# Packing with products for pairs of heads, loads per pair, a split moved into the softmax, and another order of q's turns, in a fused attention and feed-forward kernel on one core

## What is computed

```python
def sm_attn(qq, kk, vv):
    s = scale * np.matmul(qq, kk.transpose(0, 1, 3, 2))
    s = s - np.max(s, axis=-1, keepdims=True)
    a = np.exp(s)
    a = a / (np.sum(a, axis=-1, keepdims=True) + 1e-09)
    return np.matmul(a, vv)
p_packed = sm_attn(p, k, v)
out = sm_attn(q, p_packed, p_packed)
# x = out as (4608, 512); then
h = x @ w_in                       # 512 to 1024
solu = h * softmax(h)
ln = (solu - mean(solu)) / sqrt(var(solu) + 1e-06) * g_ln
x = ln @ w_out                     # 1024 to 512
h = maximum(maximum(x @ w1, x @ w2), x @ w3)
return h @ w_out2
```

## Time and profile before

| | |
|---|---|
| median of three runs | 1071.45 us (1068.35 to 1072.98) |
| profiled execution | 1070.61 us |
| its span, first to last instruction | 1068.8 us |
| mean granted TensorE clock | 0.977 of full speed |
| TensorE busy | 1014.4 us, 95% |
| VectorE, ScalarE, GpSimd busy | 605.5, 344.5, 250.8 us (57%, 32%, 23%) |
| TensorE busy in slices of 26.7 us | 0.7 to 0.8 in the first eight, 0.9 and more from then on |

### The profile page before, as it was taken

The page is one execution under the profiler, slowest core; times in us unless marked ns, Lnnn a source line. Parts: engine busy times, 40 slices in busy tenths (PEclk is TensorE's granted clock), DMA queues, the critical chain, the costliest instruction groups (busy, mean ns, idle before and its releaser), DMA issues.

```text
span 1068.8 us, 16036 instructions
## 1 busy us (share of the span) xinstructions
PE 1014.4 (95%) x6626; PEld 813.0 (76%) x6626; DVE 605.5 (57%) x980; ACT 344.5 (32%) x551; POOL 250.8 (23%) x222
## 2 busy tenths in 40 slices
PE   7878876999999999999999999999999999999998
PEld 5544543778888888888888888888888888888887
DVE  2776756785666567756456553656365643663021
ACT  4645533243343243233322142223322241223111
POOL 0223553285794669360000000000000000000000
PEclk9889987999999999999999999999999999999999
DMA  7867851434644446123565535454355535542341
GB/s 247 308 227 274 286 173 63 163 99 160 216 163 159 145 153 239 79 119 109 204 259 206 177 110 213 172 184 176 137 184 205 206 109 187 206 142 86 117 159 40
DMA packets 46633, 183.24 MB, mean 171 GB/s; under 512 B 7520, under 2 KB 7520, under 8 KB 36960
## 3 DMA queue, kind: packets, MB, share of 16 engines
q1 hardware_dynamic: 40336, 147.20, 38.6%
q0 software_dynamic: 6224, 35.00, 9.0%
HBM read 134.62 MB, written 47.58 MB: 170 GB/s over the span
## 4 chain that ended last, share of the span: by engine, by line
PE 82%; DVE 8%; issue 4%; ACT 3%; DMA 2%; POOL 1%; ACTq 0%; POOLq 0%
PE ps L1082 27%; PE ps L716 25%; PE ps L1114 14%; PE ps L1105 5%; PE ps L730 3%; PE ps L983 2%; PE ps L865 1%; PE ps L822 1%; DVE h_lo L1473 1%; PE ps L774 1%; DVE spot L1770 1%; DMA q_raw<-in_q_dram 1%; PE ps L732 1%; DVE spot L1761 1%; DVE bn L1657 1%
## 5 line engine op out<-in xcount | busy, mean ns | idle before, releaser
L1082 PE MATMUL ps<-ys,slot 128*128 128x512 f32 x1512 | 345.7, 390 | 0.5
L1082 PEld LDWEIGHTS ps<-ys,slot 128*128 128x128 f32 x1512 | 283.2, 188 | 62.5 <-ACT spot L1157 3.9
L1761 DVE TENSOR_TENSOR spot<-ps,spot 128x512 f32<-128x512 f32 x108 | 74.3, 688 | 99.2 <-PE ps L1082 73.7
L1157 ACT ACTIVATE spot<-ps 128x512 f32<-128x512 f32 x90 | 52.8, 596 | 207.5 <-PE ps L1082 196.4
L716 PE MATMUL ps<-ln_hi,w_out_s_lo 128*128 128x512 f32 x280 | 109.0, 389 | 0.0
L716 PE MATMUL ps<-ln_lo,w_out_s_hi 128*128 128x512 f32 x280 | 108.9, 389 | 0.0
L716 PE MATMUL ps<-ln_hi,w_out_s_hi 128*128 128x512 f32 x280 | 108.9, 389 | 0.0
L1114 PE MATMUL ps<-w_out_s_lo,h_hi 128*128 128x512 f32 x216 | 84.0, 389 | 0.0
L1114 PE MATMUL ps<-w_out_s_hi,h_hi 128*128 128x512 f32 x216 | 84.0, 389 | 0.0
L1114 PE MATMUL ps<-w_out_s_hi,h_lo 128*128 128x512 f32 x216 | 84.0, 389 | 0.0
L1288 ACT ACTIVATE u<-ps,neg_max 128x1024 f32<-128x1024 f32 x36 | 40.2, 1116 | 125.4 <-DVE neg_max L1639 125.4
(11 more groups left out here) (152 smaller groups left out, 1476.0 us busy)
## 6 DMA issues: line engine op xcount, KB each, us to landing
slot<-w_operands SPq DMA_DIRECT2D x36, 1792.0 KB, 7.2
w_operands<-stage POOLq DMA_DIRECT2D x18, 1024.0 KB, 4.9
k_raw<-in_k_dram SPq DMA_DIRECT2D x16, 576.0 KB, 5.1
v_raw<-in_v_dram SPq DMA_DIRECT2D x8, 1152.0 KB, 7.7
q_raw<-in_q_dram SPq DMA_DIRECT2D x8, 1152.0 KB, 8.1
y_features<-yst SPq DMA_DIRECT2D x9, 1024.0 KB, 4.5
y_raw<-y_features SPq DMA_DIRECT2D x9, 1024.0 KB, 5.3
out_dram<-spot SPq DMA_DIRECT2D x36, 256.0 KB, 2.1
```

What stands on the lines that cost most here:

```text
L1082: last = pe.matmul(ps[:, group_bank(g, k), :], w[:, a - 1, i, kk, :], ys[:, b, j, kk, :], start=n < 4 and kk == 0 and e == 0, stop=kk == K ...
L1157: return act.activation(dst, src, ACT.Copy)
L1761: dve.tensor_tensor(dst[:, :], a, b, op).then_inc(ready, 1)
```

## The change

- `pack`: instead of one product for each head, one for each pair of heads: 64 columns of `a1T` (two heads' packed rows) by 128 columns of `v_raw` (two heads' features). Of each result two of four 32x64 blocks are of use. 36 products instead of 72 for a batch.
- `take_packed` scales 128 different columns instead of writing 64 twice; `copy_packedT` picks the useful blocks in four copies; `packedT` has one place for each head, and its two memsets go.
- `k_raw` and `q_raw` are loaded in four transfers each, one for each slot (a pair of heads, one of each half), each waiting only for the turns of its slot. The ninth tokens (QH) are turned first in q, and in k from batch 1 on; so the first turn of a batch needs all four transfers.
- TensorE: `turn_q(b+1, 2)` stands ahead of `merge(b)`, the turns 3 and 4 right behind it, ahead of `scores1(b+2, 0)`. VectorE: `copy_q(b+1, 2)` stands ahead of both `turn_out`.
- `centre(n)` moves on VectorE from the end of the step to between `max2(b, 1)` and `inverse2(b, 0)`; `split_w_out` is cut into `hi_w_out`, between `sub2` and `scale2`, and `lo_w_out`, behind `scale2` and ahead of the stores.

```diff
-                for x in range(2):
-                    at = slice(2 * x, 2 * x + 2)
-                    sp.dma_start(k_raw[:, at, :, :].rearrange("p h j d -> p h (j d)"), k_v[b][:, at, :])\
-                        .then_inc(k_loaded[x], 16)
+                for h in range(QH):
+                    if b > 0:
+                        sp.wait_ge(kT_filled, (QH + 1) * (b - 1) + (QH + 1 if b == 1 else h + 2))
+                    sp.dma_start(k_raw[:, h, :, :].rearrange("p j d -> p (j d)"), k_v[b][:, h, :])\
+                        .then_inc(k_loaded[h], 16)
...
-                if b > 0:
-                    sp.wait_ge(qT_filled, (QH + 1) * b)
-                sp.dma_start(q_raw[:, :, :, :].rearrange("p h j d -> p h (j d)"), q_v[b]).then_inc(q_loaded, 16)
+                for h in range(QH):
+                    if b > 0:
+                        sp.wait_ge(qT_filled, (QH + 1) * (b - 1) + h + 2)
+                    sp.dma_start(q_raw[:, h, :, :].rearrange("p j d -> p (j d)"), q_v[b][:, h, :]).then_inc(q_loaded, 16)
...
             for b in range(B - 1):
                 for g in range(QUADS):
                     sub2(b, g)
+                if b > MEAN_STEP:
+                    hi_w_out(b - MEAN_STEP - 1)
                 for g in range(QUADS):
                     scale2(b, g)
+                if b > MEAN_STEP:
+                    lo_w_out(b - MEAN_STEP - 1)
                 if b >= 2:
                     store_weights(b)
                     store_merged(b)
-                if b > MEAN_STEP:
-                    split_w_out(b - MEAN_STEP - 1)
...
-                    for h in range(QH):
-                        rows = slice(h * NPACK, (h + 1) * NPACK)
+                    for x in range(2):
+                        rows = slice(x * 2 * NPACK, (x + 1) * 2 * NPACK)
                         for g in range(QUADS):
-                            last = pe.matmul(ps[rows, u_banks[g], 0:D], a1T[half(g), m, rows],
-                                             v_raw[half(g), h, token_of(m), :], start=m == 0, stop=m == J - 1)
+                            last = pe.matmul(ps[rows, u_banks[g], 0:2 * D], a1T[half(g), m, rows],
+                                             v_raw[half(g), 2 * x:2 * x + 2, token_of(m), :], start=m == 0, stop=m == J - 1)
...
+                if second:
+                    turn_q(b + 1, 2)
                 if third and first:
                     merge(b)
                 if second:
-                    turn_q(b + 1, 2)
+                    turn_q(b + 1, 3)
+                    turn_q(b + 1, QH)
                 if first:
                     scores1(b + 2, 0)
-                if second:
-                    turn_q(b + 1, 3)
-                    turn_q(b + 1, QH)
...
-                for jj in range(2):
-                    part = slice(jj * D, (jj + 1) * D)
-                    last = dve.tensor_copy(packedT[b % 2][part, :, 1 - jj, :], src[part, :, :])
+                src = turned("packed", b)[:, 0:QUADS * P].rearrange("c (y l n) -> c l y n", l=2, n=NPACK)
+                dst = packedT[b % 2][:, :, :].rearrange("c (y l) n -> c l y n", l=2)
+                for l in range(2):
+                    for jj in range(2):
+                        last = dve.tensor_copy(dst[half(jj), l], src[half(l), l])
...
                     max2(b, 1)
+                if third and MEAN_STEP < b <= MEAN_STEP + K1 // 2:
+                    centre(b - MEAN_STEP - 1)
+                if third:
                     inverse2(b, 0)
...
                     copy_packedT(b + 1)
+                if second:
+                    copy_q(b + 1, 2)
                 if third:
                     turn_out(b, 0)
```

More of the change, by code:

```diff
@@ L170, in packed_attention_ffn @@
     column_mean = place("column_mean", [P, DM])
-    packedT = [place(f"packedT{i}", [P, H, 2, NPACK]) for i in range(2)]
+    packedT = [place(f"packedT{i}", [P, H, NPACK]) for i in range(2)]
     assert cursor[0] <= small_base
@@ L222, in packed_attention_ffn @@
     w_in_loaded = sem("w_in_loaded")
-    k_loaded = [sem(f"k_loaded{i}") for i in range(2)]
+    k_loaded = [sem(f"k_loaded{i}") for i in range(QH)]
     v_loaded, q_loaded, p_loaded = sem("v_loaded"), sem("q_loaded"), sem("p_loaded")
@@ L326, in tokens_ones, with k_order @@
         return t[:, :, :].rearrange("c g (p j) -> c g j p", j=J)[:, :, J - 1, :]
+    def k_order(b):
+        return (0, 1, 2, 3, QH) if b == 0 else (QH, 0, 1, 2, 3)
+    Q_ORDER = (QH, 0, 1, 2, 3)
     def first_col(b):
@@ L750, in column_means, with turn_k @@
                 pe.matmul(bank[:, :], share[:, :], column_part[:, :], start=True, stop=True).then_inc(mean_filled, 1)
-            def turn_k(b, j):
-                bank = take_bank("k", b, j)
-                if j % 2 == 0:
-                    pe.wait_ge(k_loaded[min(j // 2, 1)], 16 * b + 16)
-                turn_rows(bank, k_raw, j).then_inc(kT_filled, 1)
+            def turn_k(b, n):
+                bank = take_bank("k", b, n)
+                x = k_order(b)[n]
+                for h in range(QH) if x == QH else (x,):
+                    pe.wait_ge(k_loaded[h], 16 * b + 16)
+                turn_rows(bank, k_raw, x).then_inc(kT_filled, 1)
             def turn_p(b):
@@ L1608, in step @@
                     turn_out(b, 1)
-                if second:
-                    copy_q(b + 1, 2)
                 if direct:
@@ L1617, in step @@
                     lo_a(b)
-                if third and MEAN_STEP < b <= MEAN_STEP + K1 // 2:
-                    centre(b - MEAN_STEP - 1)
                 if third and not first:
```

70 lines of the change are left out of this document (36 added, 34 removed).

## The result

The changed kernel takes 1064.0 us (median of four runs, 1062.5 to 1064.3) against 1071.5 before: a ratio of 0.9933, with an interval from 0.9912 to 0.9953. It is 7.5 us faster where 17 were forecast; the time lies near the upper end of the range. The profiled execution took 1062.5 us, the fastest of the four, its span 1060.7.

A forecast was written before the change was run, and what follows sets the result against it. TensorE, busy 95% of the span, was taken as the bound, with gains only before about 206 us. Terms of -22.5 us at full clock and +6 for clock falls gave -16.5: 1054 to 1055 us, range 1045 to 1066.

The forecast's parts named there:

- Pack: Packing products in the attention batches: 36 wide products take 2.0 us instead of 1.66, +0.35 us a batch with copies.
- the fourth rival: In pack, 64x64 tiles don't stream side by side: 1069 us two at a time, 1100 one at a time; chance 0.06.
- The idle time inside pack: Stalls before matmuls in pack and merging, 13.3 us together, are waits for code blocks and go with fewer records.
- q's turns: Attention steps: `copy_q(2)` no longer waits for transposes, but merge comes 3.2 us later; next to nothing gained in step 3.
- sum at full clock: Step-by-step changes up to the entry without clock falls: total -22.5 us; steps 2 to 5: -0.7, +1.4, -2.3, -2.2.
- the term for the clock: 2.0 us idle ahead of q2 lowers TensorE's clock, 2.0 us a fall, three of steps 1 to 5: +6 us.
- step 6 and the entry: Last attention step into the first blocks: merge some 7 us earlier, last split out of the way; turn 13 us earlier.
- w_out: `centre` inside the softmax costs 0.3 + 0.6 us; 5.2 us leave GpSimd ahead of `sub2`; steps 4 and 5 17.0 each.
- Steps 0 and 1: First two attention steps: `copy_q(2)` leaves the way of `lo_m`, a 4.56 us stall goes; -2.1 and -4.7 us.
- The loads: Loads by head pair: the first turn up to 1 us earlier, batch 1 waits for four pieces; +0.5 us taken.
- the turn of 196.17 us: TensorE turn at the entry into the first blocks: 13 us earlier (10 to 14.5) at full clock, at about 180.
- The third rival: In the attention steps the clock falls in all five and 2 us of code waits remain: 1060 us; chance 0.19.

The follow-up runs named there:

- the order alone: Kernel before with only q2 ahead of `merge`, q3 and q4 behind it, and `copy_q(2)` early: 1079.2 us, ratio 1.0072.
- the last kernel above: Changed kernel plus six unused identity products ahead of q2, `centre` at the step's end, both split halves one step later: 1054.1 us, ratio 0.9845.
- the kernel with six products: Changed kernel, order kept, plus six identity products with unused results ahead of q2 in each step: 1055.7 us, ratio 0.9855.

## Why the prediction was right in direction and wrong in size

**Pack: right.** 2.19 and 2.20 us in seven batches, 2.60 in the eighth, for the 2.0 taken (1.92 to 2.16 was the range from rows), so +0.5 instead of +0.35 a batch. The four 64x64 tiles do run side by side; the fourth rival, which alone had the other sign, is out. The Trainium skill (TensorEngine Tiling (Array Packing), Key Properties) says they run in parallel, and the 2.2 us agree.

**The idle time inside pack: right.** No such stall stands in after; the pack of 2.60 us has a pause of 0.28 us in its weight loads, 1.5 us after a packet of code has landed. The stalls come back in all four kernels with narrow packing, at multiples of about 250 records (746, 1249 and 1993 above, and 499 with the order alone), each behind a packet of code. That the edit brings 3 us in this kernel and 9 with `merge` first is not explained by their length alone, as said there. The Trainium skill's "mostly hidden" (Runtime: NRT & Kernel Launch, Instruction fetch mechanics) isn't what these runs show: 0.3 to 4.6 us a crossing in dense stretches.

**q's turns: the step that failed.** The prediction had the mechanism whole: `merge` 3.2 us later, 2.0 us of idle ahead of q2 and the clock's fall. Its sum at full clock for steps 2 to 5 holds, as the last kernel above shows, in which `centre` is out of the way (together 0.7 us under the sum). What it mis-sized is the term for the clock. It took three falls in steps 1 to 5 at 2.0 us, +6, because in steps 3 to 5 the gap would be split into 1.0 and 1.4 to 1.6 us. It was split, into 1.76 and 1.65, and the clock fell in every step from 1 to 5 and once more on the `merge` of step 6, which the term didn't count. Against the kernel with six products, at full clock in the same stretches, the falls cost 1.5, 1.4, 1.5, 2.2 and 2.2 us in steps 1 to 5, and 2.5 in step 6 and the entry: 11.3 us for 6. The trace before couldn't carry the choice: its wait of 1.42 us, read as one that stands ahead of no fall, lies inside a stretch that is already at 1.2 GHz (40.8 to 47.6 us). And part of it is chance, since the same waits stand ahead of a fall in one trace and of none in another; the fall in step 6 is such a case. The prediction also didn't price the two halves of the edit apart, so it didn't see that with `merge` first the changed kernel is 14.8 us faster.

**w_out: the mechanism right, its price too low.** `sub2` stands right behind `max2`, `hi` delays nothing, as worked out (`scale2` ends at 124.17 us in step 4, `turn_out` starts at 124.62 behind `copy_q(2)`), and the last split no longer holds the entry: it came 12.1 us earlier for 13. But `centre` was priced at 0.3 + 0.6 us a step over its old place. Beside `sub2` it takes 0.9 us more and delays `sub2` by 0.4; by the steps at full clock the place costs 0.6 to 1.0 us a step more than the sum had (18.9, 17.8, 18.2 against 18.3, 17.0, 17.2), together 2.4, and 1.1 a step more than a place one step on. The row that could have warned was cited and used too mildly: small VectorE operations last two to three times as long while GpSimd works.

**Steps 0 and 1: right to about 1 us.** Step 0, without a fall in after, takes 19.6 us for 18.7; step 1 takes 21.1, of which 1.5 are its fall and 0.4 the pause in its pack, for 18.9. I let `copy_q(2)` leave the way of `lo_m` and looked no further; `lo_m` then was late next, with two waits of 1.5 us.

**The loads: right within what can be measured**, no gain and no loss; the start moved by +1.55 us for +1.1.

**The books at the turn of 196.17 us.** The full-clock sum put it at 173.7 us, the forecast with +6 at 179.7; it came at 188.0, 8.3 later. The clock makes 5.3 of that (11.3 for 6). `centre`'s place in steps 3 to 5 makes 2.4, steps 0 and 1 make 1.6, the start 0.4 and step 2 0.3; step 6 and the entry without that fall came 1.7 us earlier than the sum. The third rival (the clock falls in all steps, 1060) named the right cause with another rest: its code waits aren't there, the collision of `centre` is.

Between after and the kernel with six products lie 8.3 us in the medians, 8.4 at the turn and 6.7 in the two profiled spans. The 1.7 us between turn and end are the fall behind the turn shown above, which after doesn't have. Open: the value of `centre`'s place in the median, which lies between 0 and 3 us; when the same waits bring a fall of the clock and when not; and the two halves of the edit on q's turns at equal stalls.

## What to carry to other kernels

Where an engine in order waits for a buffer, look at what stood in that wait before: work that filled it for nothing costs time once it stands behind it (6.5 us here for six `merge`s of 1.95), and on TensorE the clock on top. Time two halves of an order edit apart, since here one gained and the other lost more, and read them in a step without other disturbances. If small gaps can't be closed, a few products without use in them can pay: they were worth 8 us in one place and 4.5 in three others.

## What the hardware showed unexpectedly

- **TensorE's clock after short waits.** Two waits of 1.6 to 1.8 us with 0.4 us of work between them were followed by windows of 6 and 7 us at 1.2 GHz (0.50 to 0.52 granted). `merge` went from 1.95 to 3.67 us. It isn't certain: waits of 1.49 and 1.55 us stand ahead of a fall in one trace and of none in another, and so does one of 2.27 us.
- **VectorE and GpSimd block each other.** Two VectorE operations of two f32 inputs (128x512) took 2.31 us beside a GpSimd subtraction of 128x576 and 1.41 without, the subtraction 1.60 and 1.16. The shortest, median and longest of the two, in ns:

```profile
L1495 DVE SCALAR_TENSOR_TENSOR weight_raw<-w_out_raw,gain,column_mean x2: 742/1194/1647, 116.8 to 117.4; 128x512 f32<-128x512 f32 x2
```

  The first takes 0.74 us as it does alone (to 117.50); the subtraction, begun at 116.92, ends at 118.52, some 1.0 us after it; the second ends at 119.07, 0.55 after the subtraction. The Trainium skill (SBUF — State Buffer, Who interferes with whom) has an exclusive lock on a shared pair of ports, for which a VectorE instruction with two inputs in SBUF contends with a GpSimd instruction that reads SBUF. The rows agree: the three run nearly one after another, in 2.31 us where they sum to 2.57 alone.
- **Code comes in blocks that can be felt.** A matmul with nothing to wait for stood idle for 0.3 to 4.6 us, at multiples of about 250 TensorE records, only in dense stretches, and always until 1.2 to 1.6 us after a 16 KB packet of instructions had landed. With half the instructions in the densest loop what was left is one stall of 1.01 us in one kernel and a pause of 0.28 us in another.
